# Expert network behind an attention stage: the state tile loaded by rows, zero products at the start, two folds of the lead-in on GpSimd, a second softmax over four steps

## The reference

```python
scores = scale * (x @ state^T); a = softmax(scores)          # 512 x 32 per head
xread = a @ state                                            # 512 x 64
a2 = softmax(scale * (state @ x^T)); sread = a2 @ x          # 32 x 64
rows = concat([xread, sread])  -> 4352 tokens x 512
y = ((rows @ w_a) * (rows @ w_b)) @ w_out                    # 512 -> 1536 -> 512
e = argmax(y @ w_gate); gate = softmax(y @ w_gate)[e]
out = gate * (relu(y @ w1[e]) @ w2[e])                       # 8 experts, 512 -> 1024 -> 512
```

## Time and profile before

| | us |
|---|---|
| median of three runs | 1369.45 |
| lowest and highest of them | 1368.83, 1372.33 |
| the profiled execution, its time | 1373.96 |
| the profiled execution, its span | 1371.9 |
| TensorE's matmuls busy in it | 1333.6 (97%) |
| VectorE, ScalarE, GpSimd busy | 598.7, 513.5, 381.4 |
| mean granted clock of TensorE | 0.984 of 2.4 GHz |

### The profile page before, as it was taken

The page is one execution under the profiler, slowest core; times in us unless marked ns, Lnnn a source line. Parts: engine busy times, 40 slices in busy tenths (PEclk is TensorE's granted clock), DMA queues, the critical chain, the costliest instruction groups (busy, mean ns, idle before and its releaser), DMA issues.

```text
span 1371.9 us, 20514 instructions
## 1 busy us (share of the span) xinstructions
PE 1333.6 (97%) x6730; PEld 1106.1 (81%) x6731; DVE 598.7 (44%) x1061; ACT 513.5 (37%) x880; POOL 381.4 (28%) x368
## 2 busy tenths in 40 slices
PE   7899999999999999999999999999999999999996
PEld 5678888888888888778888898887787888888884
DVE  4565476665675754766656564311111111111110
ACT  4553354543554624536433312222222222222221
POOL 1312153442444423444333301211111111111110
PEclk8999999999999999999999999999999999999998
DMA  6131455555445544554467447515778781451100
GB/s 203 55 99 50 144 162 175 157 160 172 145 159 177 156 143 147 163 167 145 142 200 250 167 134 249 193 46 162 255 242 257 246 253 74 135 194 46 38 25 1
DMA packets 129105, 208.79 MB, mean 152 GB/s; under 512 B 47688, under 2 KB 49736, under 8 KB 129032
## 3 DMA queue, kind: packets, MB, share of 16 engines
q1 hardware_dynamic: 85328, 148.03, 34.0%
q10 hardware_dynamic: 37152, 40.25, 9.9%
q0 software_dynamic: 6560, 19.67, 4.3%
HBM read 155.99 MB, written 54.26 MB: 153 GB/s over the span
## 4 chain that ended last, share of the span: by engine, by line
PE 89%; DVE 4%; DMA 2%; ACT 2%; issue 1%; POOL 1%; ACTq 0%; SPq 0%; DVEq 0%; POOLq 0%
PE YB L1520 19%; PE HB L1482 16%; PE OB L1495 16%; PE BB L1456 10%; PE AB L1456 10%; PE FB L1415 3%; PE HT L1504 2%; PE FB L1401 2%; PE FB L1330 2%; PE FB L1386 2%; DVE SW L914 2%; PE XB L1468 1%; PE FB L1411 1%; PE FB L1395 1%; DMA WS<-in_moe_w 1%
## 5 line engine op out<-in xcount | busy, mean ns | idle before, releaser
L553 POOL TENSOR_TENSOR raw<-raw,upper 128x512 f32<-128x512 f32 x128 | 167.6, 1310 | 247.7 <-DVE upper L932 247.7
L1482 PE MATMUL HB<-WS,xgh 128*128 x656 | 211.8, 404 | 4.9 <-DMA WS<-in_moe_w 2.6
L1495 PE MATMUL OB<-WS,hth 128*128 x656 | 207.5, 397 | 2.8 <-DVE htl L1225 2.8
L1520 PE MATMUL YB<-WOh,gh 128*128 128x512 f32 x408 | 165.8, 406 | 0.0
L1520 PE MATMUL YB<-WOh,gl 128*128 128x512 f32 x408 | 160.5, 393 | 0.0
L1456 PE MATMUL BB<-ATh,SW 128*128 128x512 f32 (+1 forms) x476 | 158.8, 383 | 1.7 <-DVE gl L1058 1.5
L1520 PE MATMUL YB<-WOl,gh 128*128 128x512 f32 x408 | 160.0, 392 | 0.0
L1456 PE MATMUL AB<-ATh,SW 128*128 128x512 f32 (+1 forms) x476 | 159.2, 383 | 0.0
L1225 DVE TENSOR_TENSOR htl<-HT,hth 128x1024 fp32r<-128x1024 f32 x41 | 50.2, 1225 | 241.3 <-ACT hth L787 241.3
L1482 PEld LDWEIGHTS HB<-WS,xgh 128*128 128x128 f32 x656 | 122.0, 191 | 31.6 <-issue 5.8
L914 DVE TENSOR_TENSOR SW<-FB,SW 64x512 fp32r<-64x512 f32 x176 | 121.2, 688 | 52.8 <-ACT SW L712 49.2
(11 more groups left out here) (243 smaller groups left out, 2112.4 us busy)
## 6 DMA issues: line engine op xcount, KB each, us to landing
raw<-in_moe_w SPq DMA_DIRECT2D x128, 256.0 KB, 3.1
expert_lows<-raw SPq DMA_DIRECT2D x128, 256.0 KB, 2.1
WS<-in_moe_w SPq DMA_DIRECT2D x64, 512.0 KB
WS<-expert_lows SPq DMA_DIRECT2D x64, 512.0 KB
wr<-in_moe_w_b ACTq DMA_DIRECT2D x52, 256.0 KB, 2.8
wr<-in_moe_w_a ACTq DMA_DIRECT2D x49, 256.0 KB, 3.1
y_rows<-y_sb ACTq DMA_DIRECT2D x32, 256.0 KB, 3.4
xq<-in_x SPq DMA_DIRECT2D x32, 128.0 KB, 3.2
```

Of the source, the lines that this page charges most:

```text
L553: eng.tensor_tensor(piece, piece, upper[:, :].bitcast(F32), ALU.subtract).then_inc(s["e_lo"], 1)
L1482: last = eng.matmul(HB[:, i, :], act[:, k, :], w, start=(k == 0 and m == 0), stop=(k == KC - 1 and m == 2))
L1495: last = eng.matmul(OB[:, :], act[:, k, :], w, start=(k == 0 and m == 0), stop=(k == FEC - 1 and m == 2))
L1520: last = eng.matmul(YB[:, tt, :], act[:, f % 2, c], wt[:, f, :], start=(f == 0 and i == 0), stop=(f == FC - 1 and i == 2))
```

## The change

- The state of a pair of batches is loaded as it lies: a tile `Srow` of 64 partitions (2 batches x 32 rows) by 512, with two DMAs of 64 KB, waiting for nothing at the start. TensorE turns it in four transposes of 64 columns. It is spread into its blocks when leaving PSUM (`turned_state`): three copies for each half of 64 partitions. At the start ScalarE does one half (three activations) and VectorE the other (three copies, new semaphore `st_odd`); for the later pairs ScalarE does all six for `st` and six for `sth`, VectorE six subtractions for `stl`. `st`, `sth` and `stl` are cleared once at the start, with `gp`, by four memsets on VectorE.
- SyncE, ahead of the load of a later state, now waits itself for the end of the batch before (`atl_ready`); GpSimd's clearing is gone.
- The state is the first fill, ahead of x. In place of 16 transposes of the identity TensorE runs two full-width products of zeros (`gp` with itself, 128x512) ahead of it and one behind it.
- `BY_POOL` is (0, 1): GpSimd takes the remainder of the first two folds instead of the fourth, sixth and eighth. ScalarE and VectorE do the lead-in in another order to go with it: the scores' copies come later, both turned attentions ahead of the fifth fold.
- Batch 0's second softmax starts at step 0 place 2 and takes places up to step 2 place 4 (before: step 0 place 0 to step 2 place 2, with both `s2` in step 0). The folds behind it start one place later, and end at (7, 3) instead of (7, 1). Batch 1's first two fills of x move to (3, 2) and (3, 4).

```diff
     x_v = x.rearrange("b h (p t) d -> b h p t d", t=TS)
-    state_v = state.rearrange("(q r) (g c i) n d -> r c i n q g d", r=2, c=2, i=2)
+    state_v = state.rearrange("(q r) h n d -> r n q h d", r=2)
     w_v = [w.rearrange("(k p) (j c) -> j k p c", p=P, c=512) for w in (w_a, w_b)]
...
                       (1, 1): ("yt", 2), (1, 2): ("lg", 2), (1, 3): ("yt", 3), (2, 0): ("lg", 3)}
-        BEGIN = {(0, 0): ("s2", 0), (0, 2): ("s2", 1), (1, 0): ("a2t", 0), (1, 2): ("sr", 0),
-                 (2, 0): ("a2t", 1), (2, 2): ("sr", 1)}
+        BEGIN = {(0, 2): ("s2", 0), (1, 2): ("a2t", 0), (1, 4): ("s2", 1),
+                 (2, 0): ("sr", 0), (2, 2): ("a2t", 1), (2, 4): ("sr", 1)}
+        LATER = {(2, 4): (3, 2), (3, 2): (3, 4)}
         NORM = {(6, 4): 0, (10, 2): 1}
-        FOLD_BEGIN = ((0, 1), (0, 3), (1, 1), (1, 3), (2, 1), (2, 3), (3, 0), (3, 1),
-                      (3, 3), (4, 1), (4, 3), (5, 1), (5, 3), (6, 1), (6, 3), (7, 1))
+        FOLD_BEGIN = ((0, 3), (1, 1), (1, 3), (2, 1), (2, 3), (3, 0), (3, 1), (3, 3),
+                      (4, 1), (4, 3), (5, 1), (5, 3), (6, 1), (6, 3), (7, 1), (7, 3))
         FOLD_ODD = ((4, 1), (4, 3), (5, 1), (5, 3), (6, 1), (6, 3), (7, 1), (8, 1), (9, 1), (9, 3), (10, 2), (10, 4))
...
-        PRE = (("xt", 0, 0), ("xt", 1, 0), ("st", 0, 0), ("xt", 2, 0), ("xt", 3, 0), ("a1t", 0, 0), ("a1t", 1, 0))
-        BY_POOL = (3, 5, 7)
-        WARM = 16
+        PRE = (("st", 0, 0), ("xt", 0, 0), ("xt", 1, 0), ("xt", 2, 0), ("xt", 3, 0), ("a1t", 0, 0), ("a1t", 1, 0))
+        BY_POOL = (0, 1)
...
             if b < B - 1:
-                t |= {k: (*v, b + 1) for k, v in HEADS.items()}
+                t |= {LATER.get(k, k) if b == 0 else k: (*v, b + 1) for k, v in HEADS.items()}
                 if b % 2:
...
         def load_state(eng, q):
-            eng.wait_ge(s["zero_ready"], q + 1)
-            v = Sbd[:, :, :].rearrange("n (g c) m -> n g c m", c=2)
-            for at in range(2):
-                for i in range(2):
-                    n = 64 * at + N * i
-                    for c in range(2):
-                        eng.dma_start(v[n:n + N, :, c, i * D:i * D + D], state_v[at ^ c, c, i, :, q])\
-                           .then_inc(s["state_in"], 16)
+            for r in range(2):
+                eng.dma_start(Srow[N * r:N * r + N, :, :].rearrange("n k (i d) -> n (k i) d", i=2), state_v[r, :, q])\
+                   .then_inc(s["state_in"], 16)
...
             return first_attn[:, g, :] if b == 0 else s1g[:, g, :]
+        def turned_state(tile, bank, i):
+            p = slice(D * i, D * i + D)
+            dst = tile[p, :, :].rearrange("p (g c) (a i n) -> p g c a i n", c=2, a=2, i=2)[:, :, :, :, i, :]
+            src = bank[p, 0:2 * N * KC].rearrange("p (g c a n) -> p g c a n", g=G, c=2, a=2)
+            return [(dst[:, :, 0, :, :], src[:, :, 0, :, :]), (dst[:, :, 1, 0, :], src[:, :, 1, 1, :]),
+                    (dst[:, :, 1, 1, :], src[:, :, 1, 0, :])]
...
                     if f == 0 and b % 2 and b < B - 1:
+                        eng.wait_ge(s["atl_ready"], b * 2 + 2)
                         load_state(eng, b // 2 + 1)
...
         def _(eng):
-            eng.memset(Sbd[:, :, :], 0.0).then_inc(s["zero_ready"], 1)
             eng.memset(ident[:, :], 0.0).then_inc(s["ident_ready"], 1)
...
                     constants()
-                if b % 2 and b < B - 1:
-                    eng.wait_ge(s["atl_ready"], b * 2 + 2)
-                    eng.memset(Sbd[:, :, :], 0.0).then_inc(s["zero_ready"], 1)
                 for f in range(FC):
...
                 if kind == "st":
+                    if a == 0:
+                        eng.wait_ge(s["zero_ready"], 2)
+                    if a == 1:
+                        eng.wait_ge(s["zero_ready"], 4)
                     eng.wait_ge(s["fill_done"], n + 1)
-                    eng.activation(st[:, :, :], bank.rearrange("p (a b) -> p a b", a=KC), ACT.Copy)\
-                       .then_inc(s["st_ready"], 1)
+                    for i in range(2 if a else 1):
+                        for dst, src in turned_state(st, bank, i):
+                            last = eng.activation(dst, src, ACT.Copy)
+                    last.then_inc(s["st_ready"], 1)
                     if a:
-                        eng.activation(sth[:, :, :], bank.rearrange("p (a b) -> p a b", a=KC), ACT.Copy)\
-                           .then_inc(s["sth_ready"], 1)
+                        for i in range(2):
+                            for dst, src in turned_state(sth, bank, i):
+                                last = eng.activation(dst, src, ACT.Copy)
+                        last.then_inc(s["sth_ready"], 1)
                 if kind == "xt":
...
             evac(*PRE[0], 0)
-            evac(*PRE[2], 2)
+            evac(*PRE[1], 1)
             evac(*PRE[3], 3)
...
             exp1(0, 1)
+            high_first(1)
+            evac(*PRE[5], 5)
+            high_first(2)
+            evac(*PRE[6], 6)
+            high_first(3)
             copy_scores(0)
             copy_scores(1)
-            high_first(1)
-            high_first(2)
-            evac(*PRE[5], 5)
-            high_first(3)
-            evac(*PRE[6], 6)
             for a in range(4, 8):
...
                     eng.wait_ge(s["sth_ready"], a)
-                    eng.tensor_tensor(stl[:, :, :], bank.rearrange("p (a b) -> p a b", a=KC),
-                                      sth[:, :, :].bitcast(F32), ALU.subtract).then_inc(s["stl_ready"], 1)
+                    for i in range(2):
+                        for (dst, src), (high, _) in zip(turned_state(stl, bank, i), turned_state(sth, bank, i)):
+                            last = eng.tensor_tensor(dst, src, high.bitcast(F32), ALU.subtract)
+                    last.then_inc(s["stl_ready"], 1)
                 if kind == "s1":
...
             def emit():
-                take_odd(1, 1)
+                eng.memset(gp[:, :], 0.0).then_inc(s["zero_ready"], 1)
+                eng.memset(st[:, :, :], 0.0).then_inc(s["zero_ready"], 1)
+                eng.memset(sth[:, :, :].bitcast(F32), 0.0).then_inc(s["zero_ready"], 1)
+                eng.memset(stl[:, :, :].bitcast(F32), 0.0).then_inc(s["zero_ready"], 1)
+                eng.wait_ge(s["zero_ready"], 2)
+                eng.wait_ge(s["fill_done"], 1)
+                for dst, src in turned_state(st, FB[:, 0, :], 1):
+                    last = eng.tensor_copy(dst, src)
+                last.then_inc(s["st_odd"], 1)
+                take_odd(1, 2)
                 take_odd(3, 4)
...
                 norm1(0, 0)
-                low_folded(0, YB[:, 0, :])
                 norm1(0, 1)
-                low_folded(1, YB[:, 1, :])
                 evac(*PRE[5], 5)
...
                 evac(*PRE[6], 6)
-                low_folded(4, YB[:, 0, :])
-                low_folded(6, YB[:, 2, :])
+                for a in range(3, 8):
+                    low_folded(a, YB[:, a % TS, :])
...
                 eng.wait_ge(s["st_ready"], 1)
+                eng.wait_ge(s["st_odd"], 1)
                 for a in (2 * g, 2 * g + 1):
...
                 for _ in range(n):
-                    eng.transpose(BB[:, 0:P], ident[:, :], ident[:, :])
+                    eng.matmul(BB[:, :], gp[:, 0:P], gp[:, :], start=True, stop=True)
...
                     eng.wait_ge(s[name], value)
+                    if ORDER[n - 2] == ("st", 0, 0):
+                        eng.wait_ge(s["st_odd"], 1)
                 xq, xt, s1, turned, _ = buffers(b, a // 2 if kind == "xt" else a % 2)
...
                 if kind == "st":
-                    eng.wait_ge(s["state_in"], a * 128 + 128)
-                    for c in range(KC):
-                        last = eng.transpose(bank[:, c * P:c * P + P], Sbd[:, c, :], ident[:, :])
+                    eng.wait_ge(s["state_in"], a * 32 + 32)
+                    for k in range(KC):
+                        last = eng.transpose(bank[:, 2 * N * k:2 * N * k + 2 * N], Srow[:, k, :], ident[0:2 * N, 0:2 * N])
                 if kind == "xt":
...
+            eng.wait_ge(s["zero_ready"], 1)
+            warm(2)
             eng.wait_ge(s["ident_ready"], 2)
-            warm(WARM)
-            for n in range(3):
-                fill(*PRE[n], n)
+            fill(*PRE[0], 0)
+            warm(1)
+            fill(*PRE[1], 1)
+            fill(*PRE[2], 2)
             first_scores(0)
...
                 fold_first(a)
-            fill(*PRE[5], 5)
-            fold_first(4)
-            fill(*PRE[6], 6)
-            for a in range(5, 8):
+            for n in (5, 6):
+                fill(*PRE[n], n)
+            for a in range(4, 8):
                 fold_first(a)
```

4 lines of the change are left out of this document (2 added, 2 removed).

## The result

The changed kernel takes **1362.82 us** (median of 8 runs, 1360.7 to 1364.06), the kernel before on the same chip 1371.2 (8 runs, 1366.64 to 1376.65): ratio 0.9938, 95% interval 0.9921 to 0.9956, 8.4 us faster. A second set of runs, on another chip, gives 0.9935. The profiled execution took 1363.51 us.

The account below looks back on a forecast made before the run. TensorE was taken as the bound (89% of the chain), losing time in a half-clock lead-in. Step 1 11.4 us earlier, less 1.6 moved work and 0.3 waits, gave 9.5 off 1369.45: 1360.0 us, range 1357.0 to 1366.5.

Parts of the forecast that it names:

- The state first: At the start: loading and turning the state ahead of x starts the first scores at 9.2 instead of 10.79, 1.6 us.
- The clock: Lead-in: zero products release TensorE's clock by about 6 and it stays, so ScalarE's first fold comes 5.2 us earlier.
- ScalarE's stretch and `begin`: End of lead-in: ScalarE's stretch takes 14.5 us, GpSimd's remainders are hidden, step 1's `AB` starts at 33.5 instead of 44.88.
- Work moved and waits: Batch 0 behind step 1's start: one `s2` fill and one fold moved there cost 1.6 us, waits for `FB` banks 0.3.
- the lead is handed back: Rival, batch 0: six `BEGIN` pieces each wait 1 us, so 6 to 7 of 9.5 go back; 1366.5 us, chance 0.12.
- The later three states: Later states: the chain to `gl` grows by 2.5 us under a cover of 3.3 before `BB`, so costs nothing.
- The falling clock: Rival, lead-in: the clock falls at 9.5 as before, gain only 4.6, 1364.8 us; chance 0.25, wholly or in part.
- Zeros that do nothing: Rival, start: products of zeros don't release the clock, 1366 us; counted with the rival of the clock falling as before.
- The dear copies: Rival, state's spread copies: priced like 64x512 rows, 592 and about 690 ns, 6.0 us lost per later state; 1379, chance 0.05.

Follow-up runs that it names:

- a_ident16: The changed kernel with 16 transposes of the identity ahead of the state in place of the three zero products; 1370.14 us, ratio 0.999 to the kernel before.
- a_early: The changed kernel with ScalarE's function table loaded ahead of its wait and `gp` cleared ahead of the identity wait; 1363.46 us, ratio 0.9921 to before.
- b_rows: The kernel before with only the state's part of the change (loaded by rows, first in line, spread when leaving PSUM); 1371.58 us, ratio 0.9978.
- a_no_third: The changed kernel without the third zero product, the one between the state and x; 1367.92 us, ratio 0.9959 to the kernel before.
- b_zeros: The kernel before with only its warming changed: two zero products at the start, one between first x and state; 1365.25 us, ratio 0.9946.
- a_long_spread: The changed kernel with every spread copy and subtraction of the three later states made twice; 1378.97 us, ratio 1.0063 to the kernel before.

## Why the prediction was right, and where its terms were off

The forecast was 1360.0 in 1357.0 to 1366.5, the result 1362.82. Of the 2.8 us between them 1.75 are the reference itself, 1371.2 by 8 runs where the three shown gave 1369.45. The gain was forecast as 9.5 and is 8.4.

*The state first (1.6 us).* It was 0.68. The state's DMAs had landed before TensorE was free of the zero products (a_ident16 turns the state at 5.21 without a wait), which ran until 6.04, not to 5.1: they start at 2.26, not at 1.4, since the clearing of `gp` stood behind the identity (a_early takes 0.90 of this back). The table load fell between 6.75 and 8.04, as foreseen behind the wait, and x covered even less of it. The copies were cheaper than I took them, 0.49 for three instead of 0.72. (The issue of a DMA, 4.91 / 8, is 0.61 and not the 0.64 that I wrote; nothing hangs on it.) What it is worth by itself is not settled: b_rows has 0.99 of it at the scores and nothing left at the third state in its slowest execution, and some 3 us by the ratio.

*The clock (5.2 us).* Right in mechanism and size: of the 5.78 by which the first fold is copied earlier, all but the state's 0.68 is the clock's, 5.1. The scores took 1.97 and 1.97, the second x 1.04, and ScalarE's first fold came at 16.76 (forecast 15.7, late by the 0.9 of the step above and 0.2 more). Shown by both directions: the three products out, 5.35 us lost at the third state; the three in alone, 4.29 gained. The release came later than the 6 that I wrote, within the third product, near 7 (1.35 us, for 1.12 at full clock and 1.85 at half). What I had not seen is how near it is: I gave the third product half a sentence, and without it the clock falls. Nor did it have to be zeros there; eight transposes do as well.

*ScalarE's stretch and `begin`.* The stretch until `w_out` is rounded took 31.65 - 16.76 = 14.9 (14.5). GpSimd's remainders, 5.88 from 18.67, were hidden as forecast; VectorE's last remainder, which I had at 29.3, ended at 31.6: ScalarE had come 1.1 later, and VectorE's ten last remainders stand in a row without a gap from 24.75 (6.82 together), so here VectorE and not ScalarE is the bound. The last group began at 31.83 (29.4 forecast), the clock stayed at 1.00, and step 1 began at 33.50 as forecast, but by two errors of opposite sign: the last group was 2.4 late, and no half-clock stretch followed, for which I had taken most of the way from 31.6 to 34. That the mark was met to the digit is luck.

*Work moved and waits (-1.6 and -0.3).* It was -2.63 until the first later state. TensorE's waits from step 1 to the first later state in the changed kernel, us in total, times, longest:

```profile
PE FB L1383 <- DVE SW L923: 0.3, 1, 0.3
PE FB L1348 <- DVE SW L923: 0.3, 1, 0.3
PE FB L1432 <- DVE SW L923: 0.2, 1, 0.2
```

0.8 together; before there were two of 0.3 behind the mark. So the rival in which the lead is handed back by such waits is out, the waits are 0.2 more, near the 0.3 forecast, and the work moved behind the mark is 2.4 instead of 1.6; which piece the further 0.8 is was not taken apart. For the 0.26 that each later pair of batches is longer I had nothing in the sum. Most of it stands around the turning of the state: from the last product of `ATl` ahead of it (512.23) to the next step's first `AB` (519.18) it is 6.95 us, where it was 6.74 before (520.55 to 527.29), 0.21 more. Of this 0.09 lies directly ahead of the four transposes of `Srow`, and 0.05 at the fill that needs the logits' bank.

*The later three states (0, "a cover of 3.3, 0.8 to spare").* The term was right and its argument wrong. I had looked at `BB` of the next step, the last that waits for the chain, and not at the fills, which wait for banks of `FB` that the same chain empties. The cover was 1.38. With the 2.5 us that I gave the spread copies, 1.1 would have been lost at each of three states. It held because the copies cost 0.165 each in a row, 2.0 for twelve, and the subtractions 0.19, 1.14 for six: 1.4 more than before, no more. That is luck: with the true cover the copies would cost TensorE time from a mean of (1.9 + 1.38) / 18 = 0.18 us each, not 0.29, and they came at (2.0 + 1.14) / 18 = 0.174.

*The rivals.* The falling clock was the near one: it is what a_no_third does, third state at 518.24. Zeros that do nothing are out by b_zeros. The dear copies were out at 0.165 us; a_long_spread shows that the mechanism is real, and steeper than I wrote: with 0.06 of cover left, each us by which the chain gets longer costs TensorE nearly as much.
